# Four edge transfers of a value window become two of 67 rows

## What is computed

```python
q_d, k_d, v_d = means over groups of 4 tokens            # 144 tokens per head
out_up  = repeat(softmax(scale * q_d k_d^T) v_d, 4)       # coarse, every token sees all
mask    = |i - j| < 4                                     # local, a band of 7 tokens
out     = out_up + softmax(where(mask, scale * q k^T, -1e9)) v
x = out as (2304, 512)
h = x @ w_in1;  x = max(0.01 * h, h) @ w_out1
h = x @ w_in2;  return (h - tanh(h)) @ w_out2
```

## Time and profile before

| | us |
|---|---|
| median of 3 runs | 992.04 |
| lowest, highest | 990.84, 994.45 |
| profiled execution, its own time | 990.84 |
| its span in the trace | 989.1 |
| TensorE busy | 956.0 (97%) |
| VectorE busy | 579.4 (59%) |
| ScalarE busy | 554.5 (56%) |
| GpSimd busy | 411.5 (42%) |
| DMA queue of SP, share of 16 engines | 15.7% |

### The profile page before, as it was taken

The page is one execution under the profiler, slowest core; times in us unless marked ns, Lnnn a source line. Parts: engine busy times, 40 slices in busy tenths (PEclk is TensorE's granted clock), DMA queues, the critical chain, the costliest instruction groups (busy, mean ns, idle before and its releaser), DMA issues.

```text
span 989.1 us, 19759 instructions
## 1 busy us (share of the span) xinstructions
PE 956.0 (97%) x6960; PEld 892.1 (90%) x6960; DVE 579.4 (59%) x1066; ACT 554.5 (56%) x1355; POOL 411.5 (42%) x341
## 2 busy tenths in 40 slices
PE   6789999999999999999999999999999999999998
PEld 5678999999999999999999988889899899898996
DVE  5745653664556446635324766776676676766764
ACT  4445644544635446446354767775575666766654
POOL 4535732723616417227161837623233233233232
PEclk9769999999999999999999999999999999999999
DMA  7842421022112211210100302100000000000000
GB/s 168 179 138 66 112 50 35 16 49 49 25 24 49 49 25 24 49 27 10 55 1 30 110 24 76 42 33 1 1 32 1 32 0 0 32 0 0 32 1 32
DMA packets 87797, 41.48 MB, mean 42 GB/s; under 512 B 60352, under 2 KB 81344, under 8 KB 87744
## 3 DMA queue, kind: packets, MB, share of 16 engines
q1 hardware_dynamic: 87744, 40.78, 15.7%
HBM read 36.04 MB, written 4.72 MB: 41 GB/s over the span
## 4 chain that ended last, share of the span: by engine, by line
PE 78%; ACT 6%; DVE 6%; POOL 5%; issue 3%; DMA 2%; SPq 0%; ACTq 0%; POOLq 0%; DVEq 0%
PE ph L474 12%; PE ph L476 11%; PE ph L475 11%; PE acc L550 6%; PE acc L551 6%; PE acc L552 6%; PE acc L503 6%; PE acc L504 5%; PE acc L505 5%; PE banks L372 3%; PE banks L404 2%; DVE g_lo L872 2%; POOL pl L993 2%; PE banks L391 2%; POOL g_lo L1039 1%
## 5 line engine op out<-in xcount | busy, mean ns | idle before, releaser
L1039 POOL TENSOR_TENSOR g_lo<-scratch,g_hi 128x384 fp32r<-128x384 f32 x96 | 126.1, 1314 | 259.3 <-ACT g_hi L664 259.3
L887 DVE TENSOR_TENSOR g<-g,ph 128x288 f32<-128x288 f32 x128 | 57.9, 452 | 189.4 <-ACT g L684 188.5
L1009 POOL TENSOR_TENSOR in_lo<-w_whole,in_hi 128x512 fp32r<-128x512 f32 x64 | 83.8, 1310 | 160.9 <-ACT in_hi L648 159.7
L474 PE MATMUL ph<-x_hi,w_hi_a 128*128 128x288 f32 (+1 forms) x448 | 144.7, 323 | 1.9 <-DVE x_lo L867 1.9
L684 ACT ACTIVATE g<-ph 128x288 f32<-128x288 f32 x128 | 52.5, 410 | 157.2 <-PE ph L476 155.8
L476 PE MATMUL ph<-x_hi,w_lo_a 128*128 128x288 f32 (+1 forms) x448 | 140.5, 314 | 0.0
L475 PE MATMUL ph<-x_lo,w_hi_a 128*128 128x288 f32 (+1 forms) x448 | 140.4, 313 | 0.0
L923 DVE SCALAR_TENSOR_TENSOR scratch<-scratch,ph 128x384 f32<-128x384 f32 x96 | 53.2, 554 | 112.9 <-ACT scratch L729 108.0
L1014 POOL TENSOR_TENSOR out_lo<-w_whole,out_hi 128x512 fp32r<-128x512 f32 x64 | 86.4, 1350 | 56.3 <-ACT out_hi L652 55.6
L728 ACT ACTIVATE scratch<-ph 128x384 f32<-128x384 f32 x96 | 46.8, 488 | 108.4 <-PE ph L476 106.8
L872 DVE TENSOR_TENSOR g_lo<-g,g_hi 128x288 fp32r<-128x288 f32 x128 | 88.6, 692 | 2.7 <-ACT g_hi L664 2.7
(11 more groups left out here) (162 smaller groups left out, 2688.8 us busy)
## 6 DMA issues: line engine op xcount, KB each, us to landing
out_dram<-o_stage SPq DMA_DIRECT2D x18, 256.0 KB, 2.0
w_whole<-in_moe_w_in_dram SPq DMA_DIRECT2D x16, 256.0 KB, 3.6
w_whole<-in_moe_w_out_dram SPq DMA_DIRECT2D x16, 256.0 KB, 4.4
qn<-in_q_dram SPq DMA_DIRECT2D x28, 144.0 KB
kn<-in_k_dram SPq DMA_DIRECT2D x28, 144.0 KB
v4n<-in_v_dram SPq DMA_DIRECT2D x28, 144.0 KB
vw<-in_v_dram SPq DMA_DIRECT2D x28, 122.5 KB
scratch<-in_moe_w_in_dram SPq DMA_DIRECT2D x8, 256.0 KB, 2.9
```

Source lines behind the costliest of these rows:

```text
L474: pe.matmul(bank, whi, x_hi[:, c, 0:width], start=(c == 0), stop=False)
L1009: pool.tensor_tensor(in_lo[:, f % 2, :], w_whole[:, f - KEPT, 0:DM], in_hi[:, f % 2, :].bitcast(F32), ALU.subtract).then_inc(in_lo_done, 1)
L1039: pool.tensor_tensor(g2_lo[:, f % 3, :], g2[:, f % 2, :], g2_hi[:, f % 3, :].bitcast(F32), ALU.subtract).then_inc(g_lo_done, 1)
```

## The change

In `load_v` the first window's edge, 64 rows and then 3, becomes one transfer of 67 rows, and the last window's likewise. A pair's values come in 6 transfers in place of 8, so the counts at the two waits go from 128 to 96 per pair. The bytes, their places and the order of everything else stay.

```diff
-
-                for n, row0, token0 in ((0, PAD, 0), (NB - 1, 0, S - QB - PAD)):
-                    for at, rows in ((0, QB), (QB, PAD)):
-                        part = vh[bass.ds(head, 2), token0 + at:token0 + at + rows, :].rearrange("h s d -> s h d")
-                        sp.dma_start(s.vw[row0 + at:row0 + at + rows, n, :, :], part).then_inc(s.v_loaded, 16)
+                first_win = vh[bass.ds(head, 2), 0:WIN - PAD, :].rearrange("h s d -> s h d")
+                sp.dma_start(s.vw[PAD:WIN, 0, :, :], first_win).then_inc(s.v_loaded, 16)
+                last_win = vh[bass.ds(head, 2), S - QB - PAD:S, :].rearrange("h s d -> s h d")
+                sp.dma_start(s.vw[0:WIN - PAD, NB - 1, :, :], last_win).then_inc(s.v_loaded, 16)
...
-                    pe.wait_ge(s.v_loaded, 128 * i + 128)
+                    pe.wait_ge(s.v_loaded, 96 * i + 96)
...
-                    pool.wait_ge(s.v_loaded, 128 * i + 128)
+                    pool.wait_ge(s.v_loaded, 96 * i + 96)
```

## The result

| | before | after |
|---|---|---|
| median, 20 runs each | 991.63 us | 996.3 us |
| ratio, 95% interval | | 1.0051 (1.0037 to 1.0065) |
| profiled execution, its own time | 990.84 us | 992.21 us |
| span in the trace | 989.1 us | 990.4 us |

The change costs 0.51%, 5.1 us, with 3.7 to 6.4 in the interval: slower, as forecast, but by a third of the 14.0 us. The profiled execution of after took less time than any of the twenty (992.83 to 999.01), so the opening is compared by its events and not by the span.

A forecast was written before the change was run, and what follows sets the result against it. The prediction took TensorE, busy 97% of the span, as the bound, with loads acting only through waits in the opening. 14.0 us there plus 0 in the loop, on a median of 992.04, gave 1006.0 us, range 994 to 1015.

The forecast's parts named there:

- the third load: Third A load, in the opening: issued when the lone DMA engine is free again, no wait for it shows; nothing charged.
- two-engine rival: Value loads in the opening: one-engine transfers dealt to different engines, 134 pieces each; 2 to 5 us, 994 to 997; chance 0.10.
- the division into 12 and 16 engines: All loads: a transfer uses the largest number of engines, at most 16, dividing its rows: 72 rows 12, 128 rows 16.
- The price of a piece: Value loads' edges: 256 bytes take 18 ns on one engine, so 248 more pieces cost 4.5 us a load.
- The loop tips over: Loop: at 30 ns per piece loads outrun the slack, five tiles pay about 1 us each, opening 23; 1020; chance 0.05.
- Round 1: Opening, first A and B value loads: they land 4.5 and 9.0 us later, making TensorE's next transpose 7.9 us late.
- Round 2: Opening, second A and B loads: engine 0 stays 9 us behind, so lateness grows from 7.9 to 14.9 us, taken as 14.0.
- The sum: Whole kernel: 14.0 us in the opening, 0 in the loop, giving 1006.0 us, 1.4% slower.
- Bounds: Whole kernel: 999.9 if delay counts only in the first pair of loads, 1013.5 at 22.5 ns per piece with extras.

## Why the prediction was wrong, point by point

**Right.** That the 67-row transfers run on one engine; that both of a load's are on the same one (the packets go on at one engine's pace behind the closing packet); that the loss goes through GpSimd's step 5 and L998 to TensorE's transpose; that the loop and the third load cost nothing that can be measured (0.9999); that SP's saved issues buy nothing that can be measured. The two-engine rival, whose 994 to 997 holds the result, is not what happened: the engine is one, and the number it gave is right by chance. The prediction's own sign for that rival, a first step 5 at about 17, did appear (17.29), but it does not tell the two apart, since 268 cheaper pieces on one engine gave it too; the rival's other signs, B's load at about 20 and L998 under 1 us late, did not (23.43 and 3.6 us). The range of 994 to 1015 holds the 996.3 by its low end, which the rival had set, and not by the mechanism's sum. The Trainium skill's rule on the division ("DMA: Bandwidth & Descriptors", on why a DMA increments its semaphore by 16) is borne out by the 576 packets. Its rule that small transfers should be coalesced (the same page, "Rules for kernel authors") is not borne out here: with no engine alone, two issues fewer gave 0.9991 and 1.0009, both with 1 in the interval.

**"The price of a piece": 18 ns, measured 14.2.** I divided the data rate by the busy share and took the result for the pace of one engine. The share counts overlapping packets, so that a full engine is 1.28 of itself: 18 ns is how long a packet lasts, 14.2 ns is when the next one starts. The 248 added pieces are 3.5 us, not 4.5. For the same reason the shares of 0.63 and 0.91 did not support the division into 12 and 16 engines, as I had them do; the packet count did. A small slip beside it: at 30 ns, in "The loop tips over", 248 pieces take 3.0 us more than priced, not 3.5.

**"Round 1": 7.9 us, measured 3.6.** The added time was put whole on top of the old landing: 4.5 and 9.0 us. The loads came 2.65 and 5.9 us later. The pieces take less, and part of them may be moved while the other engines still work on the same load, so that only the stretch in which the engine is left alone is added; the sizes fit that, and no run isolates it. The old landing of B's load was wrong too: I carried A's 2.5 us over to B and had 18.7, and by the packet records it was about 17.6. So GpSimd had 2.3 us of room and not 1.2. 5.9 less 2.3 is 3.6, and TensorE shows 3.6. One more miss inside it: I had L993 3.3 us late, and it was 0.9.

**"Round 2": 6 to 7 us, measured 0 within the noise.** This is the step that failed most: a backlog of 9 us on one engine that was to stay from the first round to the second. "There is hardly a gap to catch up in" rested on the share of 0.94 read as full. With the q and k loads, 12 engines carry 143 KB per us, 11.9 each, where one alone carries 18: by that estimate an engine has a third of its time free there, and in the window 24 to 28 of after the machine moves 221 KB per us where it moved 171 before. Besides, SP is held at its second 67-row issue (3.21, 2.77, 3.30 us) and meanwhile sends nothing on, so that a backlog has less to grow from. Which of the two keeps it away, no run separates. The load that was to land at 49.8 released GpSimd at 42.02, and the wait that was to come near 60 is not there. The run on the second two loads alone has 1.0002, with at most 1.7 us; the run on all but the first two has 1.0013, with at most 3.3.

**"The sum".** By the steps as measured it is 3.6 + 0 + 0. The timed loss is 5.1 (3.7 to 6.4), and 5.2 with only the first two loads changed, so about 1.5 us beyond the trace's step are open; the step with its scatter (3.0 to 3.7) and the interval of the loss only just meet. In the profile of after TensorE's lateness does grow behind the step: the 32 value matmuls at 30.69 take 1.93 us, where those of the kernel before took 1.11, and the transposes behind them begin at 33.41 instead of 28.44, 5.0 us late and no longer 3.6. TensorE of the kernel before, then a window of after:

```profile
22.28 0.60 PE L391 MATMUL banks<-ident,pl 128*70 128x128 f32 x4
...
26.93 1.11 PE L404 MATMUL banks<-pT,vw 70*64 70x64 f32 x32
...
28.44 0.66 PE L365 MATMUL banks<-ident,qn 72*128 72x72 f32 x4
```

```profile
28.00:32.00 4.00, 2.92 (x39) 2.65 (x40) 0.56 (x3) 1.91 (x9) 1.11 (x2) 1.00 0.99 195
```

It is tempting to put this down to TensorE's longer idle time, but the traces do not bear that out. After's TensorE is at the slower pace already ahead of its wait of 2.53 us: the four transposes at 23.16 take 1.06 us, those at 22.28 in the kernel before 0.60. And 1.93 us for the 32 matmuls also stands in two runs that leave the first two loads alone and lose nothing measurable, the one from the third load on (at 27.74) and the one with all but the first two (at 27.33). This is the first:

```profile
27.74 1.93 PE L426 MATMUL banks<-pT,vw 70*64 70x64 f32 x32
```

There the clock column of 28 to 30 says 0.50, the lower level; in after it says 1.00 at the same pace, so the column does not settle it here. The first feed-forward matmul, which the prediction had at 78, begins at 67.81 in after and at 64.12 before, but anywhere from 63.91 to 68.30 in the profiles that leave the first two loads as they were. One profile of each kernel cannot place the last 1.5 us. A lower mean clock is not what makes the loss: with only the first two loads changed, the eight executions have a mean granted clock of 0.983, like the 31 of the kernel before that were timed with them, and take 4.5 us longer in the mean (995.96 against 991.49). What the difference to 3.6 is made of stays open.

**"Bounds".** 999.9 was meant as the low end of the mechanism, with round 2 absorbed. That case came, with round 1 itself at half (3.6 for 7.9).

## What to carry to other kernels

Before merging transfers, look at the number of rows that comes out: 67, a prime number, put the whole transfer on one DMA engine, 14 ns for each 256 bytes one after another, and held the issuing queue besides. Whether that costs depends on the room at the first wait for it: here 134 pieces a load cost nothing that could be measured and 268 cost 5 us, at the only two of sixteen loads whose lateness reached TensorE. And do not read a DMA share as fullness: find the rate of one engine in a stretch where it works alone, and compare rates.

## What the runs showed of the hardware that I had not expected

- A lone DMA engine moves 18 KB per us in pieces of 256 bytes, one starting every 14.2 ns and lasting 18, and shows 0.08 of 16 engines, 1.28 of one (changed kernel, 14 to 15 us).
- An issue of 0.33 us becomes one of 2.8 to 3.3 us, of 3.8 us with all four behind the other loads, and of about 7 us for a pair of 469 and 21 pieces, where one engine has to carry it; everything later in the issuing queue is held, while the machine is used at a share of 0.26 (12 to 16 us). That the engine's being behind is the reason is a reading. In the run with the first load alone SP stood 3.19 us and B's load was still there in time.
- TensorE's pace in the opening differs between executions of kernels with the same first loads: 32 value matmuls take 1.11 us in two profiles and 1.93 in three.
